# First channel product by Strassen's algorithm over pairs of hidden tiles, with token sums in PSUM

## The chip, the cores and the metric

The kernel runs on one core of one Trainium2 chip. The metric is device time in microseconds (us), from the kernel's start to its end. In what follows PE is TensorE (matmuls; PEld is its weight load), DVE is VectorE, ACT is ScalarE, POOL is GpSimd and SP is SyncE, which issues the DMAs.

## What is computed

Three layers follow one another: local attention with a few global keys, an MLP mixer over tokens and then channels, and a second mixer whose angles come from its input. The change lies in the mixer's channel products and at the border to the second mixer.

```
x = attention(q, k, v)                      # B=2, S=768 tokens, 8 heads of 64, so 512 channels
h = relu(xT @ w_tok1) @ w_tok2              # over tokens, per batch; 768 -> 256 -> 768
u = x + hT
x2 = u + relu(u @ w_ch1) @ w_ch2            # over channels; 512 -> 1536 -> 512
theta = x2 @ w_theta
y = w_tok_r @ (x2 * cos(theta)) + w_tok_i @ (x2 * sin(theta))
u2 = x2 + y
out = u2 + relu(u2 @ w_ch)
```

Everything is float32. Every product is made of three matmuls of rounded parts: an operand is split into a high part (rounded to the type that PE takes, fp32r) and the remainder, and high x high, high x low and low x high are added in PSUM (function `three`).

## The kernel before

The program is written engine by engine, with semaphores between the engines. Each engine runs its own list in order, so the order of the code of an engine is its order on the chip. The stages are: attention (to about 93 us), then for each of the two batches the token products, the channel products, and then the second mixer for both batches.

**Token products** of a batch. `hidden_tokens` makes two tiles of relu(xT w_tok1); ACT writes the high part and DVE the remainder (L1099). `mixed_tokens` makes eight pieces of 128 channels x 384 tokens in PSUM banks 0 to 5 and again 0 and 1. For each piece DVE adds x in place (L1114, semaphore u_done), ACT writes the high part of u (L799, uT_hi), and DVE writes the remainder (`lo_of_u`, L1108, uT_lo).

**Channel products.** The 1536 hidden channels are twelve tiles f of 128, the 768 tokens two halves c of 384 (SC). `hidden(i)` makes one of the 24 (c, f) pieces: four channel blocks k, three matmuls each, so 12 matmuls of 384 columns. ACT and DVE split its relu (L806, L1123). `reduce_hidden(i)` multiplies the piece with w_ch2 into four PSUM banks, 12 matmuls of 384 columns. PE alternates hidden(i) with reduce_hidden(i - 1). After each half of the tokens DVE takes the sums (`take_h2`, L1041) and adds the low part of u (`finish_x2`, L1047).

**Weights.** SP loads chunks of 1536 or 1024 columns into two raw buffers; POOL writes their high part (L650) and their remainder (L651) into ten slots. The order is the list ORDER. w_ch1 and w_ch2 are split once and stay for both batches. The six chunks of the second mixer's token weights (TOKRI) get their high part from ACT (`round_tokri`, L767), the remainder from POOL.

**Second mixer.** `angles(g)` makes the 128 x 512 angles of one tile of tokens (12 matmuls of 512 columns); it needs the split tile of x2 (`tile_to_hi` on ACT, `tile_to_lo` on DVE, L1032). `find_angles` (six DVE operations, L1056 to L1066), `sines` (ACT), `multiply_x` (L1076), `z_to_hi` (ACT) and `z_to_lo` (L1081) make the operands of `mix(g)`: 24 matmuls of 512 and 24 of 256 columns. Before, angles(0) stands among the last channel products, angles(1) behind them, and angles(g + 1) ahead of each mix(g).

## Time and profile before

| | us |
|---|---|
| median of 3 runs | 504.42 |
| lowest, highest | 504.38, 504.49 |
| profiled execution, its own time | 504.52 |
| its span (first to last instruction) | 502.7 |

The table's last two lines belong to one execution, so 1.8 us lie around the span. In a timeline a row is a run of like instructions: start, length, engine, line, operation, out<-in, shape and count, and in brackets how long the engine idled before it and what ended that. "L288" is the line of the helper `three`, so matmuls are told apart by the names of their operands. The length of a PE row reaches to the end of its last matmul, which overlaps the next row; the pitch is the distance between starts.

### The profile page before, as it was taken

The numbers are of one execution on the slowest core, as the hardware profiler recorded it, in microseconds if no ns is written. First come the engines' busy times: TensorE is split into PE (matmuls) and PEld (weight loads), VectorE is DVE, ScalarE is ACT, GpSimd is POOL, SyncE is SP. The second block draws the span as 40 slices with busy tenths as digits, with TensorE's granted clock in tenths as the row PEclk, the third lists the DMA queues.
The fourth block names the chain that finished last, engine by engine and source line by source line (L and its number), as shares of the span: only waits on it lengthen the run. The fifth ranks groups of instructions, "written<-read, shape, count | busy, mean of one in ns | idle before, by whom it ended". The sixth has DMA issues, their size and how long they took to land.

```text
span 502.7 us, 8110 instructions
## 1 busy us (share of the span) xinstructions
PE 495.9 (99%) x2977; PEld 467.6 (93%) x2977; DVE 271.4 (54%) x715; ACT 175.7 (35%) x375; POOL 141.5 (28%) x131
## 2 busy tenths in 40 slices
PE   7999999999999999999999999999999999999997
PEld 5999999899999999989999999998888899888897
DVE  6998998672212421075212424247787665764452
ACT  6999898541111111123111143422333320321130
POOL 3575666499900000005000041730320220000040
PEclk9999999999999999999999999999999999999999
DMA  7897775634431100002020212320001221000002
GB/s 236 321 310 233 234 220 138 198 125 135 158 94 31 45 2 0 1 0 86 41 60 4 60 34 96 125 84 1 1 2 48 64 78 64 1 0 1 1 33 94
DMA packets 24777, 43.50 MB, mean 87 GB/s; under 512 B 3104, under 2 KB 17440, under 8 KB 24736
## 3 DMA queue, kind: packets, MB, share of 16 engines
q1 hardware_dynamic: 24736, 42.96, 26.8%
q8 instruction: 24, 0.39, 0.3%
q14 instruction: 17, 0.14, 0.1%
HBM read 33.52 MB, written 3.15 MB: 73 GB/s over the span
## 4 chain that ended last, share of the span: by engine, by line
PE 97%; DVE 1%; DMA 1%; issue 0%; ACT 0%
PE bank L288 74%; PE bank L1456 7%; PE bank L1236 5%; PE bank L1266 4%; PE bank L1269 4%; PE bank L1250 2%; PE bank L1248 2%; DMA counts<-both_counts 1%; PE bank L1276 0%; DVE wsplit L875 0%; DVE wsplit L946 0%; DVE act_raw L1209 0%; ACT probsT L673 0%; ACT wsplit L680 0%; DVE scores L866 0%
## 5 line engine op out<-in xcount | busy, mean ns | idle before, releaser
L288 PE MATMUL bank<-hid,wsplit 128*128 128x384 f32 x576 | 109.2, 339 | 0.0
L288 PE MATMUL bank<-split,wsplit 128*128 128x384 f32 x576 | 109.0, 339 | 0.0
L288 PE MATMUL bank<-wsplit,zs 128*128 128x512 f32 (+1 forms) x576 | 103.3, 338 | 0.0
L288 PEld LDWEIGHTS bank<-wsplit,zs 128*128 128x128 f32 x576 | 89.8, 188 | 14.2
L288 PEld LDWEIGHTS bank<-hid,wsplit 128*128 128x128 f32 x576 | 102.0, 188 | 0.3 <-DVE hid L1123 0.2
L288 PEld LDWEIGHTS bank<-split,wsplit 128*128 128x128 f32 x576 | 102.1, 188 | 0.1
L1123 DVE SCALAR_TENSOR_TENSOR hid<-bank,hid 128x384 fp32r<-128x384 f32 x48 | 26.8, 558 | 134.9 <-ACT hid L806 134.9
L651 POOL TENSOR_TENSOR wsplit<-wraw,wsplit 128x1536 fp32r<-128x1536 f32 (+1 forms) x19 | 62.8, 3308 | 76.2 <-ACT wsplit L767 75.2
L806 ACT ACTIVATE hid<-bank 128x384 fp32r<-128x384 f32 x48 | 23.6, 491 | 146.7 <-PE bank L288 146.5
L650 POOL CAST wsplit<-wraw 128x1536 fp32r<-128x1536 f32 (+1 forms) x13 | 17.4, 1338 | 125.8 <-PE bank L288 117.2
L582 POOL TENSOR_TENSOR wsplit<-qk_raw,wsplit 64x256 fp32r<-64x256 f32 x46 | 38.0, 826 | 33.7 <-DVE wsplit L883 33.3
L660 POOL TENSOR_TENSOR split<-act_raw,split 128x384 fp32r<-128x384 f32 x12 | 12.5, 1071 | 109.5 <-ACT split L840 109.5
L724 ACT ACTIVATE probs<-scores,nmax 128x232 f32<-128x232 f32 (+1 forms) x96 | 39.9, 465 | 1.8 <-DVE nmax L987 1.6
L771 ACT ACTIVATE zb<-zb 128x512 f32<-128x512 f32 x12 | 7.6, 632 | 87.4 <-DVE zb L1066 87.4
L288 PE MATMUL bank<-wsplit,tile 128*128 128x512 f32 x144 | 35.6, 395 | 0.0
L987 DVE CUSTOM_DVE_ANT_0 scores<-bank,bias 128x232 f32<-128x232 f32 (+1 forms) x96 | 32.5, 375 | 5.0 <-PE bank L1236 4.1
L1236 PE MATMUL bank<-wsplit 128*128 128x232 f32 (+1 forms) x192 | 32.7, 292 | 2.2 <-DVE wsplit L875 1.2
L1456 PE MATMUL bank<-split,wsplit 128*128 128x384 f32 x192 | 33.9, 337 | 0.0
L1266 PE MATMUL bank<-vt,probsT 128*128 128x65 f32 x192 | 33.8, 264 | 0.1
L1456 PEld LDWEIGHTS bank<-split,wsplit 128*128 128x128 f32 x192 | 33.5, 188 | 0.2
L288 PEld LDWEIGHTS bank<-wsplit,tile 128*128 128x128 f32 x144 | 26.3, 188 | 5.5
L1269 PE MATMUL bank<-vt,probsT 104*128 104x65 f32 x160 | 30.9, 275 | 0.0
(104 smaller groups left out, 599.5 us busy)
## 6 DMA issues: line engine op xcount, KB each, us to landing
wraw<-weights SPq DMA_DIRECT2D x16, 768.0 KB, 4.1
qk_raw<-qk SPq DMA_DIRECT2D x23, 528.0 KB, 4.7
vt<-v SPq DMA_DIRECT2D x10, 520.0 KB, 4.5
xT<-turned SPq DMA_DIRECT2D x64, 48.0 KB, 2.0
out<-act_raw SPq DMA_DIRECT2D x16, 192.0 KB, 1.9
wraw<-weights SPq DMA_DIRECT2D x4, 512.0 KB, 3.3
xT<-turned_early SPq DMA_DIRECT2D x16, 96.0 KB, 2.5
xT<-wraw SPq DMA_DIRECT2D x32, 48.0 KB, 1.9
```

Of the source, the lines that this page charges most:

```text
L288: mm = pe.matmul(dst, lhs(a), rhs(c), start=first and i == 0, stop=last and i == 2, skip_group_check=True)
L582: pool.tensor_tensor(q_split[D:P, n % 2, heads], q_in[D:P, n % 2, heads], q_split[D:P, n % 2, heads].bitcast(F32), ALU.subtract).then_inc( ...
L650: link(pool.tensor_copy(w_at(slot, 0, 0, width), raw))
L651: pool.tensor_tensor(w_at(slot, 1, 0, width), raw, w_at(slot, 0, 0, width).bitcast(F32), ALU.subtract).then_inc(w_ready, 1)
L724: act.activation(probs[:, n % 2, h, first:], scores[:, m % 2, e, first:], ACT.Exp, bias=nmax[:, n % 2, h:h + 1], scale=-1.0).then_inc(exp_ ...
L806: act.activation(r1s[:, i % 3, 0], bank[6 + i % 2][:, 0:SC], ACT.Relu).then_inc(r1_hi, 1)
L987: dve.tensor_tensor_reduce(out=scores[:, m % 2, e, first:], in0=S_BANK[m % 2][e][:, first:WIN], in1=bias[:, h, first:], scale=-SCALE, scal ...
L1123: dve.scalar_tensor_tensor(r1s[:, i % 3, 1], bank[6 + i % 2][:, 0:SC], 0.0, r1s[:, i % 3, 0].bitcast(F32), ALU.max, ALU.subtract).then_inc ...
L1236: mm = pe.matmul(S_BANK[m % 2][e][:, first:WIN], q_split[:, n % 2, h, :], k_split[:, i, h, key:key + WIN - first], start=i == 0, stop=i == 1)
L1266: mm = pe.matmul(dst, probsT[:, m % 2, at + P:at + 2 * P], vt[:, n % 2, 0, cols], start=m % 2 == 0 and e == 0, stop=n % T == 0, skip_group ...
L1269: mm = pe.matmul(dst, probsT[0:SEEN, m % 2, at:at + P], vt[0:SEEN, n % 2, 1, cols], start=False, stop=True, skip_group_check=True)
L1456: return pe.matmul(bank[at][:, 0:SC], w_at(CHAN_AT[k_ // 2], w, k_ % 2 * DM + d * P, P), S_(u, k_, c * SC, SC), start=first, stop=last, sk ...
```

## The change

Of w_ch1 and w_ch2 the tiles f and f + 6 now form a pair; there are six pairs. Pair 0 is multiplied as before (`REGULAR`: four pieces of 12 matmuls). Pairs 1 to 5 go by one level of Strassen's algorithm (Winograd's form): channels in two halves, the two hidden tiles, the tokens in two halves. Seven products of six matmuls take the place of eight. They need

- sums of the weights: POOL makes four sums for each pair (mix_raw) and splits three quarters and four sums, for both batches anew, since only two pairs are held at a time; chunks 2 to 13 are loaded twice;
- sums of the tokens: eight pieces T1 to T4 of 384 columns, once for each batch, formed in PSUM by DVE (`find_sum`) from the banks and from copies of u (`u_raw`, six ACT copies for each batch), then split by ACT (`sum_to_hi`) and DVE (`sum_to_lo`);
- joining of the products: ACT copies the first (`p1`), DVE forms u2, u3, c22 in SBUF and two sums in banks 6 and 7, and four relu pieces for each pair are split as before.

`reduce_hidden` becomes `block`: three matmuls of 512 and three of 256 columns; the sums are kept over all 768 tokens, so `take_h2` and `finish_x2` come once for each batch, eight operations each. PE alternates a product and a block. DVE turns tiles of x for the next stage (L336, L341) in pairs 1 and 3. angles(0) stands at the start of the second batch's last pair, angles(1) after that pair's products, and angles(g + 2) ahead of mix(g). The work of DVE for angles(0) and angles(1) moves with them. The TOKRI slots and the places where ACT rounds them are new.

```diff
+            def split_first(n, raw):
...
+                a11, a12, a22, a21 = (raw[:, q * 2 * P:(q + 1) * 2 * P] for q in range(4))
+                s1, s2, s3, s4 = (mix_raw[:, q] for q in range(4))
+                link(pool.tensor_tensor(s1, a21, a22, ALU.add))
+                link(pool.tensor_tensor(s3, a11, a21, ALU.subtract))
+                link(pool.tensor_tensor(s2, s1, a11, ALU.subtract))
+                rounded(mixes(n, 0, 0, 3), raw[:, 0:3 * 2 * P])
+                link(pool.tensor_tensor(s4, a12, s2, ALU.subtract))
...
+                        if n >= 2:
+                            pool.wait_ge(r1_ready, products_by(*divmod(n - 2, PAIR_F)))
+                        if n == PAIR_F + 1:
+                            pool.wait_ge(tile_lo, 2 * T)
+                        split_first(n, raw).then_inc(w_ready, 1)
...
+                    if i < 6:
+                        act.activation(u_raw[:, i], U_BANK[i][:, 0:SC], ACT.Copy).then_inc(u_copied, 1)
...
+                for i, (f, c) in enumerate(REGULAR):
+                    if 1 <= i:
+                        find_sum(2 * i)
+                        find_sum(2 * i + 1)
+                    dve.wait_ge(r1_hi, b * PARTS + i + 1)
+                    dve.scalar_tensor_tensor(r1_at(b * PAIR_F, f, 1, c * SC, SC), bank[6 + i % 2][:, 0:SC], 0.0,
...
+                    if i == 0:
+                        sum_to_lo(1)
+                    else:
+                        sum_to_lo(2 * i)
+                        sum_to_lo(2 * i + 1)
...
             z_to_lo(0, 1)
+            find_angles(1)
+            take_h2(B - 1, 0)
+            take_h2(B - 1, 1)
+            multiply_x(1)
+            for i in range(2, 2 * KD):
+                take_h2(B - 1, i)
             tile_to_lo(B * T + 2)
-            for d in range(KD):
-                finish_x2(B - 1, NC - 1, d)
+            z_to_lo(1, 0)
+            for i in range(2 * KD):
+                finish_x2(B - 1, i)
...
+                    wait_weight(pair_in_order(b, i, 0))
+                    pe.wait_ge(r1_lo, parts - 1)
+                    product(i, 0, 6, quarter(0, 0), False)
+                    block(i - 1, *blocks[2 if ahead else 0])
+                    pe.wait_ge(p1_copied, m + 1)
+                    product(i, 1, 6, quarter(2, 0), True)
...
-                    if s + 1 < T and not (b and s == 0):
+                    if b == 0 and s + 2 < T:
+                        angles(g + 2)
+                    if b and 1 <= s < T - 1:
                         angles(g + 1)
                     mix(g)
```

DVE, in the first batch, from the last pieces of u to the first hidden tiles. Before (bank is PSUM, xT holds x, split holds u's parts, hid the hidden pieces):

```order
L1114 TENSOR_TENSOR bank<-bank,xT 128x384
L1108 TENSOR_TENSOR split<-bank,split 128x384
L1114 TENSOR_TENSOR bank<-bank,xT 128x384
L1108 TENSOR_TENSOR split<-bank,split 128x384 x2
L1123 SCALAR_TENSOR_TENSOR hid<-bank,hid 128x384 x4
```

Now (L1299 adds x, L1270 is u's remainder, L1288 is `find_sum`, L1293 `sum_to_lo`, L1316 the remainder of a hidden piece; the sums and the pieces lie in wsplit):

```order
L1270 TENSOR_TENSOR split<-bank,split 128x384 x2
L1288 TENSOR_TENSOR bank<-bank,u_raw 128x384 x2
L1299 TENSOR_TENSOR bank<-bank,xT 128x384
L1293 TENSOR_TENSOR wsplit<-bank,wsplit 128x384
L1299 TENSOR_TENSOR bank<-bank,xT 128x384
L1270 TENSOR_TENSOR split<-bank,split 128x384 x2
L1316 SCALAR_TENSOR_TENSOR wsplit<-bank,wsplit 128x384
L1293 TENSOR_TENSOR wsplit<-bank,wsplit 128x384
L1288 TENSOR_TENSOR bank<-bank,u_raw 128x384 x2
L1316 SCALAR_TENSOR_TENSOR wsplit<-bank,wsplit 128x384
L1293 TENSOR_TENSOR wsplit<-bank,wsplit 128x384 x2
```

Between two remainders of hidden pieces DVE now has three or four operations on token sums.

DVE at the start of the second batch, with the semaphores waited for. Now (L1081 is the third of three remainders of x tiles, L1202 `finish_x2` of the first batch, L1258 the hidden tokens' remainder, L1299 the first addition of x). POOL's wait for tile_lo, which the diff shows, ends with the first of these rows:

```order
L1081 TENSOR_TENSOR third<-act_raw,third 128x512 [waits tile_hi]
L1202 TENSOR_TENSOR act_raw<-act_raw,split 128x512 [waits acc_taken] x2
L1202 TENSOR_TENSOR act_raw<-act_raw,split 128x256 [waits acc_taken]
L1258 SCALAR_TENSOR_TENSOR hid<-bank,hid 128x512 [waits h1_hi] x2
L1202 TENSOR_TENSOR act_raw<-act_raw,split 128x256 [waits acc_taken]
L1202 TENSOR_TENSOR act_raw<-act_raw,split 128x512 [waits acc_taken] x2
L1202 TENSOR_TENSOR act_raw<-act_raw,split 128x256 [waits acc_taken] x2
L1299 TENSOR_TENSOR bank<-bank,xT 128x384 [waits h_ready,xT_in]
```

Before, four `finish_x2` stood there in all, two of them behind the hidden tokens.

POOL, one pair's weights (mix_raw holds the sums of weights, wraw the loaded chunk); before, two rows (L650, L651) made a chunk:

```order
L712 TENSOR_TENSOR mix_raw<-wraw 128x256
L713 TENSOR_TENSOR mix_raw<-wraw 128x256
L714 TENSOR_TENSOR mix_raw<-mix_raw,wraw 128x256
L701 CAST wsplit<-wraw 128x768
L716 TENSOR_TENSOR mix_raw<-wraw,mix_raw 128x256
L701 CAST wsplit<-mix_raw 128x1024
L704 TENSOR_TENSOR wsplit<-wraw,wsplit 128x768
L704 TENSOR_TENSOR wsplit<-mix_raw,wsplit 128x1024
L701 CAST wsplit<-wraw 128x1024
L704 TENSOR_TENSOR wsplit<-wraw,wsplit 128x1024
```

Ten operations a pair, in both batches.

## Rows read from the trace of the kernel before

**Rows 1.** The page: busy time of PE, and the chain's shares by engine.
```profile
PE 495.9 (99%) x2977; PEld 467.6 (93%) x2977; DVE 271.4 (54%) x715; ACT 175.7 (35%) x375; POOL 141.5 (28%) x131
...
PE 97%; DVE 1%; DMA 1%; issue 0%; ACT 0%
```
**Rows 2.** Waits of PE, longest line: who waited, for whom, us in total, times, longest.
```profile
PE bank L1276 <- DVE wsplit L853: 1.5, 1, 1.5
```
**Rows 3.** Timeline of PE, token and channel products and start of the second mixer.
```profile
101.85 8.72 PE L288 MATMUL bank<-wsplit,hid 128*128 128x384 f32 x48
110.40 4.40 PE L288 MATMUL bank<-split,wsplit 128*128 128x384 f32 x24
114.64 2.28 PE L288 MATMUL bank<-hid,wsplit 128*128 128x384 f32 x12
...
333.60 2.97 PE L288 MATMUL bank<-wsplit,tile 128*128 128x512 f32 x12
336.40 8.64 PE L288 MATMUL bank<-wsplit,zs 128*128 128x512 f32 x48
344.88 2.97 PE L288 MATMUL bank<-wsplit,tile 128*128 128x512 f32 x12
...
398.48 2.96 PE L288 MATMUL bank<-wsplit,tile 128*128 128x512 f32 x12
```
**Rows 4.** Groups of PE by shape: the two channel products.
```profile
L288 PE MATMUL bank<-hid,wsplit 128*128 128x384 f32 x576 | 109.2, 339 | 0.0
L288 PE MATMUL bank<-split,wsplit 128*128 128x384 f32 x576 | 109.0, 339 | 0.0
```
**Rows 5.** Timeline of DVE while u is made in the first batch.
```profile
104.84 1.03 DVE L1114 TENSOR_TENSOR bank<-bank,xT 128x384 f32<-128x384 f32 x2 [1.74 <-PE bank L288]
105.96 0.56 DVE L1108 TENSOR_TENSOR split<-bank,split 128x384 fp32r<-128x384 f32 x1
106.44 0.56 DVE L1114 TENSOR_TENSOR bank<-bank,xT 128x384 f32<-128x384 f32 x1
```
**Rows 6.** Timeline of ACT: one high part of u, and four copies in a row.
```profile
107.03 0.49 ACT L799 ACTIVATE split<-bank 128x384 fp32r<-128x384 f32 x1 [0.63 <-DVE bank L1114]
...
400.37 1.77 ACT L840 ACTIVATE split<-act_raw 128x384 fp32r<-128x384 f32 x4 [2.02 <-DVE act_raw L1182]
```
**Rows 7.** Timelines of POOL: weights split alone, copy and remainder.
```profile
69.79 0.73 POOL L611 TENSOR_TENSOR wsplit<-wraw,wsplit 128x256 fp32r<-128x256 f32 x1
...
99.14 1.47 POOL L650 CAST wsplit<-wraw 128x1536 fp32r<-128x1536 f32 x1 [7.39 <-DVE third L933]
100.69 3.50 POOL L651 TENSOR_TENSOR wsplit<-wraw,wsplit 128x1536 fp32r<-128x1536 f32 x1
...
229.70 1.04 POOL L650 CAST wsplit<-wraw 128x1024 fp32r<-128x1024 f32 x1 [90.50 <-PE bank L288]
230.82 2.40 POOL L651 TENSOR_TENSOR wsplit<-wraw,wsplit 128x1024 fp32r<-128x1024 f32 x1
```
**Rows 8.** Timelines of DVE and POOL where both read SBUF at once.
```profile
88.29 3.46 POOL L651 TENSOR_TENSOR wsplit<-wraw,wsplit 128x1536 fp32r<-128x1536 f32 x1
89.58 2.72 DVE L933 TENSOR_TENSOR tile<-act_raw,tile 128x512 fp32r<-128x512 f32 x1
...
352.99 0.81 DVE L1076 TENSOR_TENSOR zc<-xT,zc 128x512 f32<-128x512 f32 x1 [1.31 <-ACT zc L772]
353.34 2.74 POOL L651 TENSOR_TENSOR wsplit<-wraw,wsplit 128x1024 fp32r<-128x1024 f32 x1
353.73 2.90 DVE L1076 TENSOR_TENSOR zb<-xT,zb 128x512 f32<-128x512 f32 x1
```
**Rows 9.** Timeline of DVE: one tile's angles, remainders of 512 columns.
```profile
339.46 0.43 DVE L1057 TENSOR_SCALAR za<-za 128x512 f32<-128x512 f32 x1
...
345.23 0.69 DVE L1081 TENSOR_TENSOR zs<-zc,zs 128x512 fp32r<-128x512 f32 x1
345.84 0.69 DVE L1081 TENSOR_TENSOR zs<-zb,zs 128x512 fp32r<-128x512 f32 x1
```

More of the change, by code:

```diff
@@ L78, with pair_chunks, pair_in_order @@
 BORROWED = 5
-ORDER = [0, 1, 2, 6, 3, 7, 4, 8, 5, 9] + list(range(10, 20))
+def pair_chunks(first, last):
+    return [n for i in range(first, last) for n in (2 + 2 * i, 3 + 2 * i)]
+ORDER = ([TOK1, TOK2] + pair_chunks(0, PAIR_F) + pair_chunks(0, 2) + [THETA, THETA + 1]
+         + pair_chunks(2, PAIR_F) + list(range(TOKRI, CHAN + 2)))
+THETA_IN = ORDER.index(THETA)
+TOKRI_IN, CHAN_IN = ORDER.index(TOKRI), ORDER.index(CHAN)
+def pair_in_order(b, i, second):
+    return 2 + 2 * PAIR_F * b + 2 * i + second + (2 if b and i >= 2 else 0)
 BESIDE = [1, 3]
@@ L1167, in _ @@
                         z_to_lo(g, 0)
+                    if g and not (b and s == 0):
                         z_to_lo(g, 1)
@@ L1394, in _, with block @@
[L1394 to L1399 removed]
+                def block(i, f, d):
+                    n = b * PAIR_F + i
+                    first, last = i == 0 and f == 0, i == PAIR_F - 1 and f == 0
+                    if d == 0:
+                        wait_weight(pair_in_order(b, i, 1))
+                        pe.wait_ge(r1_lo, b * PARTS + 2 * NC * i + (3 + f if i == 0 else 4 - f))
+                    if first:
+                        pe.wait_ge(t_lo, b * SUMS + 5 + d)
+                        pe.wait_ge(t_raw, b * SUMS + 7 + d // 2)
+                    three(pe, bank[d][:, :], lambda a: second_at(n, a, f * DM + d * P, P),
+                          lambda a: r1_at(n, f, a, 0, 512), first, last)
+                    mm = three(pe, bank[4 + d // 2][:, d % 2 * 256:(d % 2 + 1) * 256],
+                               lambda a: second_at(n, a, f * DM + d * P, P),
+                               lambda a: r1_at(n, f, a, 512, S - 512), first and d % 2 == 0, last)
+                    mm.then_inc(h2_done, 1)
@@ new lines, in product, with quarter, summed @@
+                def product(i, mix, at, rhs, more):
+                    for kk in range(2):
+                        mm = three(pe, bank[at][:, 0:SC], lambda a: mix_at(b * PAIR_F + i, a, mix, kk),
+                                   lambda a: rhs(a, kk), kk == 0 and not more, kk == 1)
+                    mm.then_inc(r1_ready, 1)
+                def quarter(k_, c):
+                    return lambda a, kk: S_(a, k_ + kk, c * SC, SC)
+                def summed(t):
+                    return lambda a, kk: sum_at(t, kk, a)
@@ new lines, in _ @@
+                for i in range(1, PAIR_F):
+                    m = b * JOINS + i - 1
+                    parts = b * PARTS + 2 * NC * i
+                    order = (0, 1) if i == 1 else (1, 0)
+                    blocks = [(f, d) for f in order for d in range(KD)]
+                    ahead = b == B - 1 and i == PAIR_F - 1
+                    if ahead:
+                        angles(0)
+                        block(i - 1, *blocks[0])
+                        block(i - 1, *blocks[1])
+                        pe.wait_ge(th_taken, 1)
+                    wait_weight(pair_in_order(b, i, 0))
[4 more added lines that the diff above has]
+                    product(i, 1, 6, quarter(2, 0), True)
+                    block(i - 1, *blocks[3 if ahead else 1])
+                    pe.wait_ge(r1_lo, parts)
+                    pe.wait_ge(t_lo, b * SUMS + 6)
+                    product(i, 4, 7, summed(2), False)
+                    block(i - 1, *blocks[4 if ahead else 2])
+                    pe.wait_ge(r1_lo, parts + 1)
+                    product(i, 5, 6, summed(3), False)
+                    if not ahead:
+                        block(i - 1, *blocks[3])
+                    pe.wait_ge(u_taken, 3 * m + 1)
+                    product(i, 3, 7, summed(1), False)
+                    if not ahead:
+                        block(i - 1, *blocks[4])
+                    pe.wait_ge(u_taken, 3 * m + 2)
+                    pe.wait_ge(t_lo, b * SUMS + 8)
+                    product(i, 2, 6, summed(4), False)
+                    block(i - 1, *blocks[5])
+                    pe.wait_ge(u_taken, 3 * m + 3)
+                    product(i, 6, 7, quarter(2, 1), True)
+                    block(i - 1, *blocks[6])
+                    block(i - 1, *blocks[7])
@@ L1401, in _ @@
+                if b == B - 1:
+                    angles(1)
+                for d in range(KD):
+                    block(PAIR_F - 1, 1, d)
                 if b + 1 < B:
@@ L1403, in _ @@
                     hidden_tokens(b + 1, 0, 1).then_inc(tile_used, 1)
-                reduce_hidden(CHB - 1)
+                for d in range(KD):
+                    block(PAIR_F - 1, 0, d)
             def mix(g):
@@ L1409, in mix @@
                 if b == 0:
[L1410 removed]
+                    wait_weight(TOKRI_IN + s)
                 if s == 0:
```

460 lines of the change are left out of this document (306 added, 154 removed).

## Prediction

> **What bounds the kernel now.** I read the page's busy times and chain first. PE is busy in 99% of the span and holds 97% of the chain that ended last [rows 1]. The view of waits shows PE waiting 1.5 us at most, once, at the start [rows 2]; the granted clock is 1.00 throughout (2.4 GHz), so no row has PE at its lower level. The timeline of PE then gives pitches. From 110.40 to 114.64, 24 matmuls of 384 columns take 4.24 us, 176.7 ns each. From 336.40 to 344.88, 24 of 512 and 24 of 256 columns take 8.48 us, 353.3 ns a pair, the same as two of 384 [rows 3]. Work taken from PE is therefore a full gain, and any wait that it gets is a full loss. So the question is whether the other engines can follow.
>
> **1. Products removed.** The first channel product has 576 matmuls of 384 columns [rows 4]. Now there are, for each batch, 4 x 12 in pair 0 and 5 x 7 x 6 in the others, 258 instead of 288. 60 fewer in all, at 176.7 ns: **-10.6 us**. The blocks have 576 matmuls as before, half of 512 and half of 256 columns; at 353.3 ns a pair that is 0. The Trainium skill, "TensorE: Matmul & The Clock Gate", section "Back-to-back issue gap", gives columns / 2.4 + 2.5 ns for an isolated matmul, 162.5 ns here, by which the gain would be 9.8 us; the row is the measured pitch and decides.
>
> **2. Token sums at the start of each batch.** This is new work on DVE and ACT just where PE's next work depends on it. Durations: DVE's operations of 384 columns with one operand in PSUM take 0.56 us and follow each other at 0.47 us [rows 5]; ACT's take 0.49 [rows 6] and, independent, follow at 0.42 (four in 1.77, so (1.77 - 0.52) / 3, the 0.52 being one of these). From one engine's end to the other's start I add 0.035 us (105.96 follows an ACT operation begun at 105.44). [...]
>
> DVE starts at 104.84. Ahead of the first hidden remainder its list has 19 operations: 8 additions, 8 remainders, 2 token sums, 1 remainder of a sum. 19 x 0.465 = 8.8 us. Since each remainder now waits for two ACT operations (high part, copy), 1.5 us are added (0.6 at the first, 0.5 at the sixth, the rest small). So this remainder starts at 115.2 and ends at 115.8, and the third regular product, which writes the same bank, could start at 110.33 + 4.24 = 114.6: **1.25 us**. The next remainders go round in 2.9, 3.4 and 3.4 us: remainder(s) of sums, two new sums, two ACT high parts, ACT's relu, the remainder. In numbers, for the first: 3 x 0.465 + 0.56 + 0.42 + 0.49 + latencies = 2.9. A regular product takes PE only 2.12. Hence PE waits 0.8 us ahead of the fourth product, 1.3 ahead of the first Strassen product, 0.3 for the seventh sum ahead of the first block, and 0.8 for the copy p1, which stands behind the last relu in ACT's list. Together **4.4 us a batch, 8.9 in both**. After that the pairs run freely: 15 pieces of 1.06 us, 15.9 us, against 9 DVE operations (and three turns in pairs 1 and 3), and each result has three pieces to travel. POOL needs for a pair, at the linear rates through its rows [rows 7], 4 sums at 0.73, copies 0.83 + 1.04, remainders 1.85 + 2.40, seven gaps of 0.08 (100.69 less 100.61), so 9.6, then 3.5 for the second half: 13.1 of 15.9 us.
>
> **3. Start of the second batch.** Where DVE reads two operands from SBUF and POOL works, the later one stands still: the remainder at 89.58 took 2.72 instead of 0.69 us and ended 0.55 after POOL's operation; the one at 353.73 took 2.90, and POOL's at 353.34, issued while DVE held on, took 2.74 instead of 2.40. Additions with a PSUM operand beside POOL's chunk at 100.69 to 109 stay at 0.56 [rows 5, 8]. The Trainium skill says the same, and against this change, in "SBUF: State Buffer", section "Who interferes with whom": two SBUF inputs, or the two-port modes, against a GpSimd operation that reads SBUF, and the later is blocked for the whole of it. By that rule, and the trace agrees, one-operand work from PSUM, thus term 2, is spared.
>
> Now the list: POOL is released (tile_lo = 12) by exactly the DVE operation ahead of eight `finish_x2`, each with two SBUF operands. POOL then works for 9.6 us in eight operations. The two alternate, so every finish waits for one POOL operation. First, the last x tile's remainder comes after four more takes: PE waits 0.6 us. Three finishes ahead of the hidden tokens' remainder: 0.9 us more. Five behind: the last one waits for the 2.40 us remainder; the first addition of x starts 7.8 us after the token products of u instead of 2.8. PE has slack until its seventh piece of u: it waits 3.6 us there, 0.8 for the fourth remainder of u, and 0.4 more at the third regular product. **6.3 us**.
>
> **4. Last pair.** angles(0) needs a tile's remainder that POOL's copy of 1024 columns delays: 0.5 us. z's remainder is issued 0.2 us after POOL's remainder of the first TOKRI chunk (3.5 us); c22 stands behind it and the seventh product behind c22: 1.9 us. The margin is small; with the order reversed it is 0. **2.4 us**.
>
> **5. Ahead of mix(0).** PE wants angles(2), whose tile's remainder stands in DVE's list behind find_angles(1), eight takes and two multiplications. From the end of the last block: the six late takes (3.0 us) and the remainder, 3.2 us without any blocking. With it: find_angles' second operation (0.43 us [rows 9], SBUF to SBUF in a fast form) waits out the rest of the second TOKRI remainder, 2.9 us, and the tile's remainder 2.4 us for the third. 2.0 of these 5.3 fall where DVE would have waited for PE anyway: **6.5 us**.
>
> **6. The six mixes of batch 0.** Each step has 11.3 us of PE [rows 3] and some 9 us of DVE for one tile (six operations of angles, two products, three remainders). Now POOL's TOKRI remainders 4 to 6 and the four operations of the last chunks fall into this stage, and angles(g + 2) asks for th_taken early. One of angles(3) to (5) waits: 4.0 us (2 to 8, as the collisions fall). Before, only two chunks fell there, and PE did not wait.
>
> **Sum.** -10.6 + 8.9 + 6.3 + 2.4 + 6.5 + 4.0 = +17.5; rounding apart 17.4. From the end of the mixes of batch 0 (398.48 before) on the program is the same. Against the profiled execution's own time: 504.52 + 17.4 = **521.9 us**; that execution is 0.1 above the median, so nothing is added for it. The additional DMA (12 chunks of 512 KB) is hidden: each load is issued a chunk ahead, 13 us.
>
> **Rivals.**
> - *Blocking costs PE nothing* (the two engines give way to one another without a queue in front of PE). For: DVE idles 46% of the time. Against: rows 8. Then terms 2 and the unblocked parts stay: 4.4 + 5.1 + 0.5 + 3.2 = 13.2, with 0.6 for the x tile 13.8, less 10.6: +3.1, 507.6 us.
> - *DVE keeps ahead, and the kernel gets faster.* One mechanism: DVE's list at the start of each batch, and behind the last pair, is shorter than I reckon. All of terms 2 to 6 are lateness of this one engine. It decides from where PE's waits sum to less than 10.6 us; with none at all 493.9, more likely 495 to 503. Against: 19 operations at the measured pitch are longer than PE's lead even without ACT.
> - *POOL becomes the bound in the pairs.* 13.1 us of work in 15.9, but a chunk can start only when pair n - 2 is finished, so its slack is about 3 us. If sums and short copies cost 40% more than the linear rate, each of ten windows grows by 2: about 540. Rows 7 at 256 columns (0.73) speak against it.
> - *The clock falls.* Waits of 3.6 and 6.5 us are longer than any in the trace. If PE then went on at 1.2 GHz for as long as it had waited, it would lose half of 10 us: 527. The Trainium skill, "TensorE: Matmul & The Clock Gate", section "Loop structure matters more than you think", says that long gaps cost the fast clock; no row here shows it.
> - *The product count doesn't fall*: the list has 42 matmuls a pair, so this is excluded.
>
> **Chances.** Forecast with its blocking 0.58; its own range is 516 to 529: terms 4 and 6 can be 0.5 and 0 (down 6) or term 6 8.0 and the rounds of term 2 half a microsecond longer (up 7). Blocking free 0.17; DVE ahead 0.17; clock 0.05; POOL-bound 0.03. The range 506 to 529 takes in the first two and the clock case. A change of under 0.2%, about 1 us, can hardly be told from none; of the case with DVE ahead 0.03 ends there. Faster 0.14, same 0.03, slower 0.83.
>
> **What would show it.** Right: the new waits of PE in the page stand behind DVE, about 28 us in all; PE's matmuls of 384 columns are 60 fewer; at the token sums four or five waits of 0.3 to 1.7 us a batch; finishes of the second batch take 1 to 2.5 us each; a wait of 6 us ahead of angles(2). Wrong: if PE waits for POOL's weights in the pairs, if the sums' rounds are shorter than 2.9 us, or if finishes take 0.69 beside a busy POOL, then the named term falls.

## The result and the profile after

The changed kernel takes **528.63 us** (median of 4 runs, 528.24 to 528.80) against 504.46 (504.38 to 505.17, 4 runs) for the kernel before on the same chip: ratio 1.0474, 95% interval 1.0457 to 1.0490. It is slower by 24 us; forecast were 17.4. The profiled execution spans 526.7 us, against 502.7.

The page of the changed kernel: busy time of PE, the granted clock by slices, and the chain.

```profile
PE 496.6 (94%) x2917; PEld 449.6 (85%) x2917; DVE 342.2 (65%) x797; ACT 191.6 (36%) x413; POOL 246.1 (47%) x223
...
PEclk9999999999999999989999999979989999999999
...
PE 79%; DVE 14%; ACT 3%; issue 2%; DMA 1%; DVEq 0%; ACTq 0%
```

PE has 60 matmuls fewer than in [rows 1], as it should, but its busy time hasn't fallen: 496.6 us, against 495.9. So there are two losses, idle time and slower work, and the digits 8, 7, 8 of the clock line say where the second is. The waits of PE (who waited, for whom: us in total, times, longest):

```profile
PE bank L323 <- DVE tile L1180: 6.9, 2, 6.6
PE bank L323 <- DVE wsplit L1316: 4.7, 6, 1.1
PE bank L323 <- issue: 4.2, 1, 4.2
PE bank L323 <- DVE split L1270: 3.6, 1, 3.6
...
PE bank L323 <- DVE hid L1258: 0.9, 1, 0.9
...
PE bank L323 <- DVE third L1081: 0.4, 1, 0.4
```

In [rows 2] the longest was 1.5. L323 is the helper that issues each product as three matmuls. Nearly all of it is for DVE; "issue" (4.2) is angles(5), whose tile and remainders were there, and which stood for th_taken of angles(4), again DVE's. The timeline of PE, to lay beside [rows 3] (start, duration, count, and in brackets the idle time before it):

```profile
111.09 4.41 PE L323 MATMUL bank<-split,wsplit 128*128 128x384 f32 x24
116.53 2.33 PE L323 MATMUL bank<-split,wsplit 128*128 128x384 f32 x12 [1.03 <-DVE wsplit L1316]
119.34 2.35 PE L323 MATMUL bank<-split,wsplit 128*128 128x384 f32 x12 [0.48 <-DVE wsplit L1316]
122.79 1.29 PE L323 MATMUL bank<-split,wsplit 128*128 128x384 f32 x6 [1.10 <-DVE wsplit L1316]
124.19 1.30 PE L323 MATMUL bank<-wsplit 128*128 128x512 f32 x6
125.85 1.33 PE L323 MATMUL bank<-split,wsplit 128*128 128x384 f32 x6 [0.35 <-ACT joined L934]
127.01 1.22 PE L323 MATMUL bank<-wsplit 128*128 128x512 f32 x6
...
231.73 3.02 PE L323 MATMUL bank<-wsplit,hid 128*128 128x384 f32 x12 [3.62 <-DVE split L1270]
234.68 5.33 PE L323 MATMUL bank<-split,wsplit 128*128 128x384 f32 x24
240.56 2.33 PE L323 MATMUL bank<-split,wsplit 128*128 128x384 f32 x12 [0.55 <-DVE wsplit L1316]
...
329.44 1.31 PE L323 MATMUL bank<-split,wsplit 128*128 128x384 f32 x6 [1.92 <-DVE joined L1368]
...
350.61 5.49 PE L323 MATMUL bank<-wsplit,tile 128*128 128x512 f32 x12 [6.58 <-DVE tile L1180]
355.89 8.70 PE L323 MATMUL bank<-wsplit,zs 128*128 128x512 f32 x48
...
391.35 5.46 PE L323 MATMUL bank<-wsplit,tile 128*128 128x512 f32 x12 [4.21 <-issue]
...
422.22 2.96 PE L323 MATMUL bank<-wsplit,tile 128*128 128x512 f32 x12
```

The row at 329.44 is the seventh product of the last pair, called P6 below. The last row stood at 398.48 in [rows 3]: 23.7 of the 24.0 us of the spans are lost ahead of it. Start to start, a tile's angles take 2.80 us in [rows 3] (333.60 to 336.40); here angles(2) take 5.28 (350.61 to 355.89) and angles(5) 5.26 (to 396.61). The windows of these two stretches (us, then busy of PE, PEld, DVE, ACT, POOL, then the granted clock, DMA's share, GB/s):

```profile
350.40:354.00 3.60, 3.39 (x8) 2.71 (x9) 3.60 (x2) 0.00 (x0) 3.47 (x1) 0.50 0.64 218
391.30:395.00 3.70, 3.65 (x9) 2.90 (x10) 2.32 (x4) 1.24 (x2) 0.00 (x0) 0.50 0.01 2
```

The clock is granted at half there, the 1.2 GHz level, right after the two longest waits.

DVE is held up where the prediction has it, first z's remainder in the last pair, then the second operation of find_angles and the tile's remainder for angles(2):

```profile
324.96 3.96 DVE L1236 TENSOR_TENSOR zs<-zc,zs 128x512 fp32r<-128x512 f32 x1
...
336.39 3.36 DVE L1212 TENSOR_SCALAR za<-za 128x512 f32<-128x512 f32 x1
...
347.44 3.12 DVE L1180 TENSOR_TENSOR tile<-act_raw,tile 128x512 fp32r<-128x512 f32 x1
```

Alone they take 0.69 us (the remainders) and 0.43 [rows 9]; the last two are thus 2.9 and 2.4 us longer, as forecast. Now what DVE does at the start of the second batch, L1202 being `finish_x2`:

```profile
218.12 2.71 DVE L1202 TENSOR_TENSOR act_raw<-act_raw,split 128x512 f32<-128x512 f32 x3
...
221.94 7.71 DVE L1202 TENSOR_TENSOR act_raw<-act_raw,split 128x256 f32<-128x256 f32 x5
229.58 1.02 DVE L1299 TENSOR_TENSOR bank<-bank,xT 128x384 f32<-128x384 f32 x2
```

and POOL beside it:

```profile
218.37 1.03 POOL L712 TENSOR_TENSOR mix_raw<-wraw 128x256 f32<-128x256 f32 x1 [11.58 <-DVE third L1081]
...
226.94 2.43 POOL L704 TENSOR_TENSOR wsplit<-mix_raw,wsplit 128x1024 fp32r<-128x1024 f32 x1
```

Five finishes take 7.71 us, and the last ends (229.65) as POOL's remainder of 1024 columns does (229.37). The first addition of x starts 8.1 us after the token products of u (221.48); 7.8 were forecast.

### The profile page after: what moved, and what is told of

The parts are those of the page before. It is cut to its first block, busy times and chain, and to the rows that moved or that the text cites. A ratio compares the mean times of both kernels' runs of the same rounds, so it can differ in the third digit from the quotient of the medians.

```text
span 526.7 us, 8302 instructions
## 1 busy us (share of the span) xinstructions
PE 496.6 (94%) x2917; PEld 449.6 (85%) x2917; DVE 342.2 (65%) x797; ACT 191.6 (36%) x413; POOL 246.1 (47%) x223
## 4 chain that ended last, share of the span: by engine, by line
PE 79%; DVE 14%; ACT 3%; issue 2%; DMA 1%; DVEq 0%; ACTq 0%
PE bank L323 57%; PE bank L1744 6%; PE bank L1472 4%; PE bank L1502 4%; PE bank L1505 3%; PE bank L1486 2%; DVE act_raw L1202 2%; PE bank L1484 2%; DVE bank L1299 1%; DVE split L1270 1%; DVE wsplit L1293 1%; ACT wsplit L907 1%; DVE bank L1288 1%; DVE act_raw L1196 1%; DVE tile L1180 1%
## 5 line engine op out<-in xcount | busy, mean ns | idle before, releaser
L323 PE MATMUL bank<-wsplit 128*128 128x512 f32 (+2 forms) x816 | 148.9, 338 | 0.2
L323 PEld LDWEIGHTS bank<-wsplit 128*128 128x128 f32 x816 | 134.4, 188 | 14.2 <-issue 0.8
L704 POOL TENSOR_TENSOR wsplit<-wraw,wsplit 128x1024 fp32r<-128x1024 f32 (+2 forms) x35 | 88.4, 2528 | 43.4 <-ACT wsplit L874 41.1
L323 PE MATMUL bank<-wsplit,zs 128*128 128x512 f32 (+1 forms) x576 | 103.4, 339 | 0.0
L323 PEld LDWEIGHTS bank<-wsplit,zs 128*128 128x128 f32 x576 | 90.1, 189 | 14.3
L323 PE MATMUL bank<-split,wsplit 128*128 128x384 f32 x276 | 56.1, 345 | 7.4 <-DVE wsplit L1316 4.7
L323 PEld LDWEIGHTS bank<-split,wsplit 128*128 128x128 f32 x276 | 47.7, 191 | 10.3 <-issue 3.2
L701 POOL CAST wsplit<-wraw 128x1024 fp32r<-128x1024 f32 (+2 forms) x29 | 29.6, 1021 | 51.7 <-PE bank L323 42.4
L323 PE MATMUL bank<-wsplit,tile 128*128 128x512 f32 x144 | 40.7, 437 | 11.1 <-DVE tile L1180 6.9
L323 PEld LDWEIGHTS bank<-wsplit,tile 128*128 128x128 f32 x144 | 29.5, 211 | 18.2 <-DVE tile L1180 7.3
L1343 DVE SCALAR_TENSOR_TENSOR wsplit<-bank,wsplit 128x384 fp32r<-128x384 f32 x30 | 16.7, 558 | 38.5 <-ACT wsplit L943 27.3
L1744 PE MATMUL bank<-split,wsplit 128*128 128x384 f32 x192 | 34.2, 339 | 0.0
L1744 PEld LDWEIGHTS bank<-split,wsplit 128*128 128x128 f32 x192 | 33.8, 188 | 0.2
L1502 PEld LDWEIGHTS bank<-vt,probsT 128*128 128x128 f32 x192 | 28.8, 193 | 0.8 <-ACT probsT L782 0.7
```

The source lines that it names most:

```text
L323: mm = pe.matmul(dst, lhs(a), rhs(c), start=first and i == 0, stop=last and i == 2, skip_group_check=True)
L701: link(pool.tensor_copy(dst, src))
L704: return pool.tensor_tensor(dst, src, hi.bitcast(F32), ALU.subtract)
L1343: dve.scalar_tensor_tensor(r1_at(n, f, 1, off, SC), src, 0.0, r1_at(n, f, 0, off, SC).bitcast(F32), ALU.max, ALU.subtract).then_inc(r1_lo, 1)
L1502: mm = pe.matmul(dst, probsT[:, m % 2, at + P:at + 2 * P], vt[:, n % 2, 0, cols], start=m % 2 == 0 and e == 0, stop=n % T == 0, skip_group ...
L1744: return pe.matmul(bank[at][:, 0:SC], w_at(CHAN_AT[k_ // 2], w, k_ % 2 * DM + d * P, P), S_(u, k_, c * SC, SC), start=first, stop=last, sk ...
```

## The experiments

All were timed in three rounds beside the kernel before, which had a median of 504.37 to 504.42 us in them. The times are to be read against 528.63, the changed kernel. Up to 0.7 us of each difference isn't the edit's: in the changed kernel the clock is 0.50 from 12 to 14 us, in the attention, and its token products begin at 102.54 us (101.85 in [rows 3]); the profiled executions of the edited kernels have no such stretch there, and no edit touches it. Rows are from one profiled execution each, and the executions of one kernel differ by up to 3.2 us (run 4), so a sum of rows need not give the difference of two medians.

**1. Release POOL later in the second batch.**

```
                         if n == PAIR_F + 1:
-                            pool.wait_ge(tile_lo, 2 * T)
+                            pool.wait_ge(x2_done, NC * KD)
```

> One wait of GpSimd is changed: the first weights of the second batch's second pair are split when the eight finishes of VectorE are done, and no longer when the last tile remainder is (about 7 us later). Theory of the blocking port (VectorE's two-operand work stands still beside GpSimd's, which made the finishes 2.71 and 7.71 us long at 218.12 and 221.94): the 3.62 us wait at the seventh piece of u goes, and most of the 0.8 us before it; 5.1 us shorter by the waits, and a further 0.8 us because the granted clock of 0.86 and 0.79 at 231 to 240 us goes with the wait: about 522.7 us (521.5 to 524). Rival, that VectorE is late there by its own list: no change, 528.6. Second rival, that GpSimd then delivers the weights late: a wait for weights appears in the second batch and eats the gain, 527 or more.

Measured: **521.99 us** (520.95 to 522.83). DVE's five finishes, POOL's first operation, and PE's token products of u:

```profile
221.04 2.29 DVE L1202 TENSOR_TENSOR act_raw<-act_raw,split 128x256 f32<-128x256 f32 x5
```
```profile
223.50 0.74 POOL L712 TENSOR_TENSOR mix_raw<-wraw 128x256 f32<-128x256 f32 x1 [17.57 <-DVE act_raw L1202]
```
```profile
219.78 8.75 PE L323 MATMUL bank<-wsplit,hid 128*128 128x384 f32 x48
...
324.34 3.70 PE L323 MATMUL bank<-wsplit 128*128 128x512 f32 x12
```

Same five operations, 2.29 us instead of 7.71, and all 48 token products run without a break. The two rivals fall: the lateness wasn't in DVE's own list, and no wait for weights appears although POOL starts 5 us later (223.50, not 218.37). From PE's wait for the last x tile to its last one in the Strassen products of pair 1 are 26.2 us (217.39 to 243.55) instead of 31.6 (218.25 to 249.88): 5.5 us less, and 5.1 were worked out. The rest of the 6.6 us says little, since the profiled execution is the fastest of the four (520.95) and the clock moved both ways: the stretches behind angles(2) and angles(5) cost 1.6 us each instead of 2.5, but the 12 block matmuls at 324.34 took 3.5 us for 2.1 us of work, behind the same wait of 1.9 us at P6 that cost nothing in the changed kernel.

**2. Relu parts ahead of the token sums.**

```
                 for i, (f, c) in enumerate(REGULAR):
-                    if 1 <= i:
-                        sum_to_hi(2 * i)
-                        sum_to_hi(2 * i + 1)
                     act.wait_ge(r1_ready, b * PRODUCTS + i + 1)
                     act.activation(r1_at(b * PAIR_F, f, 0, c * SC, SC), bank[6 + i % 2][:, 0:SC],
                                    ACT.Relu).then_inc(r1_hi, 1)
+                    if 1 <= i:
+                        sum_to_hi(2 * i)
+                        sum_to_hi(2 * i + 1)
```

This is ScalarE's part; VectorE's sums move behind its relu remainder in the same way.

> Only the order is changed on ScalarE and VectorE beside the four ordinary products: from the second on, the relu part and its remainder come ahead of the two token sums, and not behind them. Theory that the sums hold the parts back: of the waits 1.25, 0.8, 1.3, 0.3 and 0.8 us in each batch, 0.8 and 1.3 go, the one at the first block grows from 0.3 to 1.1, the one at the next product falls to 0.35; 1.7 us shorter per batch, 3.4 in all: 525.2 us (524.3 to 526). Rival, that the sums themselves are what TensorE waits for there (they would only be late at a later product): no change, 528.6.

Measured: **525.29 us** (524.58 to 525.90); forecast were 525.2.

```profile
115.92 5.45 PE L323 MATMUL bank<-split,wsplit 128*128 128x384 f32 x30 [1.03 <-DVE wsplit L1313]
122.50 1.29 PE L323 MATMUL bank<-wsplit 128*128 128x512 f32 x6 [1.13 <-DVE bank L1288]
```

The waits ahead of the fourth product and the first Strassen product are gone, and 1.13 us stand at the first block for the seventh sum (L1288), as expected. From the first regular products on, PE needs 1.5 us less in each batch, where 1.7 were worked out (14.4 us from 110.48 to 124.92, against 15.9 from 111.09 to 127.01 in the changed kernel); 0.6 us more are the stretch at 12 to 14 us, so that the median's closeness to 525.2 is partly luck. What held PE back was the place of the parts behind the sums; with that gone, a sum is what PE waits for next. The rival of no change falls.

**3. Keep PE at work in its long waits**, with nothing else changed.

```
+            def fill(count, cols):
+                for _ in range(count):
+                    pe.matmul(bank[7][:, :], cols(P), cols(512), start=True, stop=True, skip_group_check=True)
+
+            FILLS = {2: 26, 5: 16}
+
             def angles(g):
...
+                if g in FILLS:
+                    if g == 2:
+                        pe.wait_ge(r1_lo, B * PARTS)
+                    fill(FILLS[g], lambda n: S_(0, 0, 0, n))
...
                 for i in range(KD, OUTB):
+                    if b and i == KD + 2:
+                        fill(14, lambda n: w_at(TOK2, 0, 0, n))
                     mixed_tokens(i, 0)
```

> Nothing that the result needs is changed or moved. TensorE gets extra products of 512 columns, whose results nobody reads, at the three long waits: 14 ahead of the seventh piece of u in the second batch, 26 ahead of angles(2), 16 ahead of angles(5); each batch of them is a little shorter than the wait that it fills (3.6, 6.6 and 4.2 us). Theory that the granted clock falls because TensorE stands still: the stretches at 0.86 and 0.79, and the two at 0.50, stay at 1.00; angles(2) and angles(5) take 2.8 us each again and not 5.3, and 0.8 us are gained behind the first: 5.8 us shorter, 522.8 us (522 to 524.5). Rival, that these two groups are slow for another reason (their operands, a load, the queue), so that the low clock of the record is only how the wait looks: no change, or up to 1 us slower, 528.6 to 529.6.

Measured: **523.19 us** (523.12 to 523.92), with a mean clock of 1.00 and a 9 for it in every slice of the page.

```profile
231.03 2.35 PE L323 MATMUL bank<-wsplit,hid 128*128 128x384 f32 x12 [0.48 <-DVE split L1270]
233.98 4.40 PE L323 MATMUL bank<-split,wsplit 128*128 128x384 f32 x24 [0.60 <-DVE split L1270]
...
350.00 3.06 PE L323 MATMUL bank<-wsplit,tile 128*128 128x512 f32 x12 [0.78 <-DVE tile L1180]
...
388.32 3.03 PE L323 MATMUL bank<-wsplit,tile 128*128 128x512 f32 x12 [0.56 <-issue]
```

This kernel has 56 matmuls *more* and is 5.4 us faster. Angles(2) take 2.90 us to the next start, 352.90 (5.28 in the changed kernel) and angles(5) 2.87 (5.26): the slow clock there comes from PE standing still, and 4.8 of the 5.4 us are these two. No slower operand or load is behind it. The third place taught something else. From 231.03 to 233.98 are 2.95 us, exactly as with the slow clock (231.73 to 234.68): a full-speed PE only waits 0.60 us for DVE instead. So my 0.8 us for that place were wrong, and the slow clock was free there. The remaining 0.6 us fit the stretch at 12 to 14 us. The Trainium skill ("TensorE: Matmul & The Clock Gate", section "Loop structure matters more than you think") says that long gaps cost the fast clock; the runs agree for these two gaps.

**4. Mix ahead of the later tile's angles**, PE's order alone.

```
-                    if b == 0 and s + 2 < T:
-                        angles(g + 2)
                     if b and 1 <= s < T - 1:
                         angles(g + 1)
                     mix(g)
+                    if b == 0 and s + 2 < T:
+                        angles(g + 2)
```

> On TensorE alone, each mix(g) of the first batch comes ahead of angles(g+2), as in the kernel before (where it was angles(g+1) ahead of mix(g), which is the same row of work). Theory: angles(2) then finds its tile ready, mix(0) waits some 3.5 us for the last takes, mix(3) some 3.3 us for its first half of z, and nothing else waits; 3.7 us shorter by the waits; the clock costs 2.48 and 2.46 us at the two old waits, at the new and shorter ones 0 to 0.9 each as behind the 3.6 us wait at 231.7: in all 7.0 to 8.6 us shorter, about 521 us (520 to 522.5). Rival, that the chain over VectorE and ScalarE sets the pace of the mixes whatever TensorE's order: 1 us or less gained by the waits, 526 to 528.6.

Measured: **520.50 us** (519.15 to 522.37).

```profile
347.26 8.71 PE L323 MATMUL bank<-wsplit,zs 128*128 128x512 f32 x48 [2.46 <-issue]
...
385.12 11.37 PE L323 MATMUL bank<-wsplit,zs 128*128 128x512 f32 x48 [3.78 <-DVE zs L1236]
```

The waits are 2.46 and 3.78 where 3.5 and 3.3 were worked out, and the forecast of 521 holds. But the two cost the clock unequally, 0.1 and 2.7 us (11.21 to the next start, 396.33, instead of 8.48), and 1.6 us more went to the clock behind P6, which made PE later and so shortened the first wait. So the forecast of the split was wrong, and the total met it partly by luck. The rows are those of the slowest of four executions (522.37 us at a mean clock of 0.987); the fastest took 519.15 at 0.993. The rival falls: PE's order alone is worth 8.1 us.

**5. The tile of angles(2) early.**

```
             z_to_lo(0, 1)
+            tile_to_lo(B * T + 2)
             find_angles(1)
...
-            tile_to_lo(B * T + 2)
```

Between the two places stand the eight takes and the products with x; ScalarE's high part of this tile moves ahead of the second TOKRI chunk in the same way.

> One step is moved on ScalarE and VectorE: the tile of angles(2) is rounded and its remainder found right behind the second half of the first z, ahead of find_angles(1) and of the takes, and no longer behind them. Reading of the trace (a chain over VectorE, ScalarE and GpSimd's long operations sets the pace ahead of the mixes, and TensorE's 6.6 us at angles(2) are only where it shows): angles(2) waits for nothing, mix(0) some 1.2 us, but angles(3) then waits 7.7 us for VectorE to have taken angles(2); 2.4 us longer by the waits, the clock costs as much as before at another place: 531 us (529.5 to 532). Rival, that the tile's late place is the cause of the wait: 6.6 us less 1.2, and the 2.5 us of its clock: 520.7 us.

Measured: **528.52 us** (528.29 to 530.10), no change, where 2.4 us more were expected.

```profile
363.78 4.80 PE L323 MATMUL bank<-wsplit,tile 128*128 128x512 f32 x12 [7.71 <-issue]
```

Angles(2) no longer wait, and angles(3) wait 7.71 us, as worked out (7.7). The 1.2 us that were worked out for mix(0) did not come. In this execution the clock cost some 1.5 us behind P6, so that PE was that much later, which would account for it. The wait has moved one tile on. The profiled execution is the slowest of the four, 1.3 us above the changed kernel's; the other three show no cost. Less clock lost behind the wait (1.8 us, not 2.5) and the 0.7 us above are part of that. So the rival (521) falls: the tile's late place is where the lateness shows, not where it comes from.

**6. POOL's TOKRI remainders in six pieces.**

```
-                    rest(w_at(slot, 1, 0, width), raw,
-                                   w_at(slot, 0, 0, width)).then_inc(w_ready, 1)
+                    step = width // 6 if TOKRI <= chunk < CHAN else width
+                    for at in range(0, width, step):
+                        done = rest(w_at(slot, 1, at, step), raw[:, at:at + step], w_at(slot, 0, at, step))
+                        if at + step < width:
+                            link(done)
+                    done.then_inc(w_ready, 1)
```

> GpSimd's remainders of the six TOKRI chunks are cut in six operations of 256 columns each (some 0.73 us, by the linear durations of the trace) in place of one of 1536 columns (3.5 us); nothing else is changed, and GpSimd works longer by it, 4.4 us a chunk. Theory that VectorE's two-operand operations stand still until GpSimd's current operation ends: each of them waits 0.7 us at most where it waited up to 3.2; of the waits, angles(2) falls from 6.6 to some 3.6 us, P6 of the last pair from 1.9 to 0, angles(5) from 4.2 to 3.4, and 0.5 appears at angles(3): 4.9 us shorter, and 1 to 3 us of the clock's cost at these two places go with it: 521.7 us (520.5 to 524). Rival, that it is the share of time in which GpSimd works that slows VectorE, whatever the length of its operations: no gain, and the longer work makes it 528.6 to 531 us.

Measured: **521.96 us** (521.12 to 522.28), forecast 521.7. POOL, then DVE, then PE:

```profile
324.04 5.35 POOL L704 TENSOR_TENSOR wsplit<-wraw,wsplit 128x256 fp32r<-128x256 f32 x6 [9.53 <-ACT wsplit L878]
```
```profile
324.10 1.22 DVE L1240 TENSOR_TENSOR zs<-zc,zs 128x512 fp32r<-128x512 f32 x1
```
```profile
344.57 3.06 PE L323 MATMUL bank<-wsplit,tile 128*128 128x512 f32 x12 [3.55 <-DVE tile L1184]
```

The remainder of the first z (3.96 us in the changed kernel, 0.69 alone [rows 9]) now takes 1.22, P6 of the last pair waits for nothing, and angles(2) wait 3.55 us (forecast 3.6). POOL works longer, 5.4 to 6.2 us for what took 3.5, and the kernel is 6.7 us faster. What sets DVE's delay is the length of POOL's single operation, not the share of time in which POOL works.

Two waits missed their forecasts. Angles(3) now wait 1.84 us (0.5 forecast) and angles(5) still 3.94 (3.4), so the waits shrink by 3.4 us, not by 4.9. Of the rest, 2.4 us are the clock, which no longer falls behind angles(2), and 0.8 us the stretch at 12 to 14 us; the median's closeness to the forecast is partly luck.

**7. All of it together**, with two small steps more: z's first remainder behind c22 in the last pair, and the last two sums begun a product earlier; on PE, angles(2) alone ahead of mix(0). The "early release" of the expectation is the changed wait of run 1.

> All that the readings point to together, in the changed kernel: the early release of GpSimd in the second batch; relu parts ahead of the token sums, with the last pair of sums begun ahead of the last relu remainder; GpSimd's TOKRI remainders in pieces of 256; the tile of angles(2) early, and angles(2) alone ahead of mix(0), the later ones each behind a mix; the first half of z a step later in the last pair. If the waits add up as read, those of the two product stretches fall to 2.3 and 2.8 us, the second batch's start waits 0.7, the mixes 1.4: TensorE ends the first batch's mixes 20.4 us earlier than the changed kernel did by the waits and 5 us by the clock (no wait over 2 us is left): 503 us (501.5 to 505), level with the kernel before or a little faster. Rival, that they share their gains (one chain, met at several places): 508 us or more. Second rival, that the product's saving of 10.6 us is not whole: also 508 or more, with fewer waits than that explains.

Measured: **502.96 us** (502.81 to 503.53, 7 runs): ratio to the kernel before 0.9972, 95% interval 0.9960 to 0.9983. It beats both kernels, the changed one by 25.7 us, the one before by 1.4. Its page and PE's mixes:

```profile
PE 488.1 (97%) x2917; PEld 443.9 (89%) x2917; DVE 330.7 (66%) x797; ACT 192.2 (38%) x413; POOL 255.9 (51%) x253
```
```profile
367.28 8.71 PE L323 MATMUL bank<-wsplit,zs 128*128 128x512 f32 x48 [1.00 <-DVE zs L1241]
...
388.69 8.72 PE L323 MATMUL bank<-wsplit,zs 128*128 128x512 f32 x48 [1.37 <-DVE zs L1241]
397.26 2.96 PE L323 MATMUL bank<-wsplit,tile 128*128 128x512 f32 x12
```

Against [rows 1] PE is busy 7.8 us less, with the clock at 1.00 throughout, and the last row stands 1.2 us earlier than in [rows 3]. Start to start, the waits and restarts ahead of that row still sum to 8.9 us: 2.3 and 2.8 us in the two product stretches, 0.4 at the second batch's start, 0.3 in the last pair, 3.1 in the mixes (1.4 forecast). The token products begin 0.3 us later than in [rows 3]. So the removed products gave 8.9 + 0.3 + 1.2 = 10.4 us there, of 10.6 reckoned: the saving is real, and what is left of the other terms eats most of it. Both rivals fall. One of these waits, 0.67 us at the second batch's first block, ends with POOL's weights; in the first batch PE waits as long there for a token sum.

**8. The seven edits, with the first angles out of the last pair.** PE runs angles(0) behind the last pair's products and angles(1) four blocks later; DVE and ACT do theirs behind the pair.

```
-                    ahead = b == B - 1 and i == PAIR_F - 1
+                    ahead = False
...
                 if b == B - 1:
-                    angles(1)
+                    angles(0)
                 for d in range(KD):
                     block(PAIR_F - 1, 1, d)
+                if b == B - 1:
+                    angles(1)
```

> The kernel of seven edits, with one part of the change undone: the first angles leave the last pair; angles(0) stands right behind the last pair's products, angles(1) four blocks later, and VectorE's and ScalarE's work on them behind the last pair's. It shows what that part is worth. Reading: it costs the last pair little (0.5 us and, in the changed kernel, 1.9 at P6) and spares more, since VectorE would otherwise stand before the mixes with three tiles' work: angles(2) waits 1.4 us and mix(0) 5.8 for the takes; 6.3 us longer by the waits and 1.6 to 2.7 by the clock: 511 us (509 to 512.5). Rival, that the part costs what it spares, since VectorE has the same work either way: 503 us, no change.

Measured: **512.14 us** (511.36 to 512.84), 9.2 more than kernel 7.

```profile
332.20 3.03 PE L323 MATMUL bank<-wsplit,tile 128*128 128x512 f32 x12 [1.15 <-issue]
341.11 19.07 PE L323 MATMUL bank<-wsplit,zs 128*128 128x512 f32 x96 [5.87 <-issue]
```

The waits are 1.15 and 5.87 us (1.4 and 5.8 forecast), and the clock loses 2.0 us behind the second (18.91 us to the next start, 360.02, for 16.96 of work). The rival falls, and this part of the change earns its place: it costs 2.25 us in the changed kernel and spares some 9 in a kernel whose other waits are gone.

**9. The seven edits without the pieces.** POOL's TOKRI remainders are whole again.

> The kernel of seven edits without the pieces: GpSimd's TOKRI remainders are whole operations of 1536 columns again. Reading of the blocking: VectorE stands still up to 3 us at three places of the mixes; mix(0) waits 0.7 us, mix(1) 1.1, mix(2) 0.6 and mix(3) 3.8: 5.0 us longer by the waits, and 0 to 2.7 us by the clock at the last: 509 us (507.5 to 511). Rival, that with the tile early and the order of the kernel before nothing waits for VectorE there any more: 503 to 504 us.

Measured: **510.36 us** (510.02 to 510.51), 7.4 more than kernel 7. DVE in the arithmetic of angles(3), and PE at mix(3):

```profile
360.70 3.17 DVE L1217 SCALAR_TENSOR_TENSOR zb<-za,zb 128x512 f32<-128x512 f32 x1
363.90 1.41 DVE L1219 SCALAR_TENSOR_TENSOR zc<-zb 128x512 f32<-128x512 f32 x1
365.35 2.50 DVE L1222 TENSOR_SCALAR zb<-zb 128x512 f32<-128x512 f32 x1
```
```profile
373.26 10.87 PE L323 MATMUL bank<-wsplit,zs 128*128 128x512 f32 x48 [3.92 <-DVE zs L1237]
```

Three operations of 0.69, 0.69 and 0.43 us take 7.1 us from start to end beside POOL's remainders and a copy, the one-input form of L1222 among them (2.50 instead of 0.43, [rows 9]). PE waits 3.9 us at mix(3) (3.8 forecast) and then loses 2.2 to the clock. The Trainium skill ("SBUF — State Buffer", section "Who interferes with whom") names `tensor_scalar` among the operations that can enter a two-port mode and then contend with GpSimd. That L1222, a `tensor_scalar` with one input, is held up here agrees with it. The rival falls.

## Why the prediction was near, and where it failed

The direction and the mechanism of the waits were right, and every term was within 0.6 us. The time lay 6.7 us above the point and only 0.4 us inside the range of 506 to 529. Being inside was luck: the upper end stood on a term 6 of 8.0 us and on longer rounds in term 2, and neither came. By its own steps:

1. *Products removed, -10.6.* 60 matmuls fewer. Kernel 7, start to start, gives **10.4**. The same reckoning on the changed kernel (23.7 us lost ahead of the last row, against 33.7 of waits, restarts, clock and the later start of the token products) gives 10.0.
2. *Token sums, 4.4 a batch.* Start to start, less 176.7 ns a matmul: 1.20, 0.69, 1.33, 0.34 and 0.60 us in the first batch, **4.2**; forecast were 1.25, 0.8, 1.3, 0.3, 0.8. Run 2 shows the mechanism. The second batch has 4.6, of which 0.44 are counted in term 3.
3. *Start of the second batch, 6.3.* 0.40, 0.85 and 3.62 us, then 0.83 and 0.44 more than in the first batch: **6.1**. Run 1 took the 0.85, 3.62 and 0.83 away by one wait of POOL.
4. *Last pair, 2.4.* 0.33 (the second of the two waits for a tile, 6.9 less 6.6) and 1.92: **2.25**. Run 6 removed the second by shorter POOL operations.
5. *Ahead of mix(0), 6.5.* **6.58.** Run 5 moved it, run 6 halved it. Without the blocking 3.2 were worked out: with pieces, 3.55.
6. *Mixes, 4.0.* **4.21**, at angles(5).

Together 27.5 us, less 10.6: 16.9, where 17.4 were forecast. **The step that failed is the clock.** The profile shows 4.94 us lost to it behind two waits, and run 3 gave 4.8 back. I had listed it among the rivals, with 527 us for it, but at a chance of 0.05, since no row of before had PE below 1.00. That its price was right (half of 10 us, 5) was luck: it was worked out for waits of 3.6 and 6.5 us and a slow clock as long as each wait. At the first of these the slow clock cost nothing (run 3), behind the second it cost 2.5 us, not 3.3, and the other 2.5 us came behind angles(5), which that rival did not name. To list it as a rival was a mistake of kind, not of size: the clock is no alternative to the waits, it follows from them. Once terms 5 and 6 put waits of 6.5 and 4.0 us on the path, what PE does behind them belongs into the same sum, and with the 4.9 us of the profile the forecast would have read 526.8. Of the 23.7 us ahead of the last row, 16.9 are the terms, 4.9 the clock behind these two waits and 0.7 the stretch at 12 to 14 us; of the last 1.2, 0.2 are slow clock that reaches into the mixes behind these angles, some 0.4 are restarts (each loses about 0.1, as the 2.90 for 2.80 of run 3), and 0.6 stay open.

The other rivals: blocking that costs PE nothing (507.6) is excluded by runs 1, 6 and 9. DVE keeping ahead (495 to 503) did not happen, but kernel 7 at 502.96 lies where that rival had it, after edits to DVE's and ACT's order, POOL's operations and PE's order. What stood between the change and a small gain was the lateness of DVE, mostly behind POOL, and the clock that fell with it. POOL as the bound in the pairs did not show: it needs 13 of 16 us there by the linear rates, no wait of PE in the pairs is for it, and released 5 us later (run 1) it still delivers in time.

## What to carry to other kernels

Where the bounding engine is saturated, price a change by the engines that must keep pace with it: list their operations between two of its needs, and add every wait in which a two-operand operation from SBUF, or a one-input one like L1222 from SBUF to SBUF, stands behind a long GpSimd operation. Cutting such a GpSimd operation into pieces, or starting it later, can gain although GpSimd works longer. And where a forecast puts a wait of several microseconds on TensorE, put the slow clock behind it into the sum at once, as a range (0 to 2.9 us a wait here). Giving DVE another order moved a wait by one tile and gained nothing (run 5); giving PE another order, so that it had work ready in the wait, gained 8.1 us (run 4).

## What the runs showed that I had not expected

**The clock's cost isn't set by the wait before it alone.** The table has what PE lost behind a wait, start to start against the full-speed pitch, up to the second start behind it (mix rows: up to the next start). About 0.1 of each is the restart.

| wait of PE, us | where | lost, us |
|---|---|---|
| 1.84 | run 6, angles(3) | 0.1 |
| 1.90 to 1.92 | runs 1, 2, 4 and 5, P6 of the last pair | 1.6 |
| 1.90, 1.92 | run 3 and changed kernel, same place | 0.1 |
| 2.46 | run 4, mix(0) | 0.1 |
| 2.50 | run 8, mix(3) | 0.1 |
| 3.55 | run 6, angles(2) | 0.1 |
| 3.78 | run 4, mix(3) | 2.7 |
| 3.92 | run 9, mix(3) | 2.2 |
| 3.94 | run 6, angles(5) | 2.8 |
| 4.21 | run 1, angles(5) | 1.6 |
| 4.21 | changed kernel, runs 2 and 5, angles(5) | 2.6, 2.8, 2.7 |
| 5.44 | run 1, angles(2) | 1.6 |
| 5.45 | run 2, angles(2) | 2.9 |
| 5.87 | run 8, mix(0) | 2.0 |
| 6.58 | changed kernel, angles(2) | 2.5 |
| 7.71 | run 5, angles(3) | 1.8 |

Equal waits cost 0.1 and 1.6, or 1.6 and 2.8; the longest is not the dearest. The wait of 3.62 us ahead of u's seventh piece is left out, since PE's next waits for DVE hide what the clock costs there. Each row is one execution. The edits of runs 1, 2, 4 and 5 leave P6's wait as it is, so the difference there may be one between executions rather than one of the edits; what decides stays open.

**A slow clock can be free** where the next wait is for an engine that is late anyway (run 3, 231 to 240 us), or free in part: behind P6 run 1 lost 1.6 us, and then waited 5.44 us for angles(2) instead of 6.58.
